# Layer 1 of a three-stage kernel: seven token tiles, three of them 512 wide, in place of eight of 384

## Chip, cores and metric

One Trainium2 chip, one NeuronCore. The time is that of one execution on the device in microseconds, the median of the runs shown; lower is better. A profile of one execution gives the trace.

## What is computed

A gated linear attention with a state per head, then two feed-forward layers over the same 3072 tokens (4 batches of 768), all in float32.

```python
for t in range(S):                      # B, H, S, D = 4, 8, 768, 48
    state = alpha[:, :, t, :, None] * state + einsum('bhd,bhe->bhde', k[:, :, t], v[:, :, t])
    y[:, :, t] = einsum('bhd,bhde->bhe', q[:, :, t], state)
x = y.transpose(0, 2, 1, 3).reshape(B * S, H * D)                  # 3072 x 384
x = (1 / (1 + exp(-(x @ w_gate))) * (x @ w_val)) @ w_out           # layer 1, d_ff 1536
out = maximum(maximum(x @ w1, x @ w2), x @ w3) @ w_out2            # layer 2, d_ff 768
```

## The kernel before

The program is written by hand for each engine, with semaphores between them; each engine runs its instructions in the order written.

**Layer 1** goes over tiles of tokens (`TOK` = 384, `TILES` = 8). Within a tile it goes over the 12 blocks of 128 hidden features, here called steps f = 0 to 11. A step on TensorE is `layer1` (line 1069): the gate product (`product`, lines 1020 and 1026), the value product, and the output product of the step before (`out1`, line 1045). For float32 accuracy each operand is split in a high and a low part and three of the four cross products are taken, so each of these is 3 x 3 = 9 matmuls of 128 x 128 weights against a moving operand as wide as the tile: 27 matmuls a step. ScalarE makes the sigmoid of the gate bank (`act_sb`, line 491) and the high part of h (`h_hi`, line 445), VectorE multiplies (`h_sb`, line 791) and makes the low part (`h_lo`, line 753). TensorE waits for the sigmoid before it writes the gate bank again, for h before the value bank.

**Attention** goes over 24 chunks of 128 tokens (`CH`). The first three are made ahead of layer 1; those of the tile T + 1 are made between the steps of tile T. For a chunk, VectorE runs scans of the decay factors alpha (`scans`, line 674, `decay`) and, after a reciprocal at each half chunk's end, reverse scans (`recips`, line 689, `rdec`); GpSimd scales queries and keys (`scale_qk`, lines 411 and 415); TensorE makes scores and transposes (lines 947 and 926), then outer products for the state (`outer`, line 961), and in the next step the values (`attend`, lines 994 and 976). VectorE masks the scores (`masked`, line 701), makes the next state (`new_state`, lines 724 to 729) and adds the crossed blocks (`y_add`, line 743); ScalarE copies keys (`khs_copy`), outputs (`y_copy`, line 445, into `x_raw`) and checks the range of alpha (lines 554 and 561). From the second tile on GpSimd scales; in the first, VectorE does.

The steps are fixed in the code: scans at f = 0, 3 and 6, scores at 2, 5 and 8, values at 3, 6 and 9, additions at 4, 7 and 9. On VectorE:

```python
if att and f % 3 == 0 and not scanned:
    scans(*att)
elif att and f % 3 == 2:
    masked(*att, 0)
    masked(*att, 1)
```

Before the scores TensorE waits for the last chunk's addition (`y_added`), before the outer products for both masks (`mask_done`) and the copied keys.

**Loads.** SP loads each chunk in two transfers: alpha (256 KB, line 281) and then queries, keys and values (704 KB, line 285), into one of two buffers by the chunk's parity. A buffer is free when the chunk two before has been attended and checked (`y_done`, `viol_done`). When all chunks of a tile are added, SP moves rows of the last heads into place (`move_last`, line 312). ScalarE and VectorE then split the tile's inputs (`x_hi`, `x_lo`) in step 11, for the next tile.

**Layer 2** has six tiles of 512 tokens and six steps of three products of 512 columns (27 matmuls) and an output product of 12 matmuls of 384 columns (line 1140). TensorE's layer 1 is written out tile by tile; ScalarE, VectorE, GpSimd and SP run tiles 1 to 6 in a hardware loop of two tiles a pass, three passes, so that semaphore counts are computed from a register.

## Time and profile before

| | us |
|---|---|
| median of 3 runs (850.42 to 850.93) | 850.75 |
| the profiled execution | 850.66 |
| span of its trace | 848.6 |
| TensorE busy | 838.0 |
| VectorE, ScalarE, GpSimd busy | 389.0, 280.2, 74.5 |

The span runs from the first instruction to the last end on the core; the execution's own time has some 2 us around it. Busy times of TensorE count pipelined matmuls as overlapping, so the starts tell more than the durations. The profile names a group of instructions by its line, its engine and the names it writes and reads. The rows that matter are in a section of their own below.

### The profile page before, as it was taken

How to read it: one execution, taken by the hardware profiler on the slowest of the kernel's cores; microseconds unless marked ns; L12 is line 12 of the kernel's file. 1: busy time of each engine (PE TensorE's matmuls, PEld its weight loads, DVE VectorE, ACT ScalarE, POOL GpSimd, SP SyncE). 2: the span in 40 equal slices, each digit the busy share in tenths (PEclk: the TensorE clock that was granted, in tenths of full speed). 3: DMA queues.
4: the chain of work that ended last, by engine and by line, in shares of the span. 5: the costliest groups of instructions: out<-in, count | busy, mean ns of one | idle time of the engine just before them, and what ended most of it. 6: DMA issues, size and time to landing. Idle time of an engine off the chain costs nothing.

```text
span 848.6 us, 17210 instructions
## 1 busy us (share of the span) xinstructions
PE 838.0 (99%) x6997; PEld 773.5 (91%) x6997; DVE 389.0 (46%) x959; ACT 280.2 (33%) x520; POOL 74.5 (9%) x68
## 2 busy tenths in 40 slices
PE   8999999999999999999999999999999999999997
PEld 7899999999999999999999999988888888888886
DVE  8787565555555455466465322323223232232321
ACT  4655333333333333333333334322212122221212
POOL 1000111111111011021021006300000000000000
PEclk9999999999999999999999999999999999999999
DMA  7440210210210210210200103100101001010101
GB/s 287 163 181 3 100 48 2 101 48 2 101 47 2 100 48 2 101 47 2 100 27 23 49 34 113 38 1 0 38 1 37 0 0 37 0 37 0 37 0 39
DMA packets 14461, 42.36 MB, mean 50 GB/s; under 512 B 1984, under 2 KB 5952, under 8 KB 14400
## 3 DMA queue, kind: packets, MB, share of 16 engines
q1 hardware_dynamic: 14336, 41.41, 13.7%
q8 instruction: 49, 0.80, 0.4%
q14 instruction: 12, 0.10, 0.0%
q10 hardware_dynamic: 64, 0.05, 0.0%
HBM read 35.56 MB, written 4.72 MB: 47 GB/s over the span
## 4 chain that ended last, share of the span: by engine, by line
PE 96%; DVE 2%; DMA 1%; issue 1%; ACT 0%; SPq 0%; DVEq 0%
PE ps_gv L1020 35%; PE ps_out L1045 19%; PE ps_gv L1026 18%; PE ps_out L1140 6%; PE ps_sc L1020 6%; PE ps_sc L1026 3%; PE ps_pair L1140 2%; PE ps_pair L994 1%; PE ps_pair L976 1%; PE ps_pair L926 1%; PE ps_sc L947 1%; PE ps_sc L961 1%; PE ps_pair L947 1%; DVE decay L674 0%; DVE rdec L689 0%
## 5 line engine op out<-in xcount | busy, mean ns | idle before, releaser
L1020 PE MATMUL ps_gv<-x_hi,w_hi 128*128 128x384 f32 (+1 forms) x792 | 279.8, 353 | 1.1 <-ACT x_hi L445 1.1
L1020 PE MATMUL ps_gv<-x_hi,w_lo 128*128 128x384 f32 (+1 forms) x792 | 277.2, 350 | 0.0
L1026 PE MATMUL ps_gv<-x_lo,w_hi 128*128 128x384 f32 (+1 forms) x792 | 235.1, 351 | 0.0
L1020 PEld LDWEIGHTS ps_gv<-x_hi,w_hi 128*128 128x128 f32 x792 | 148.8, 188 | 9.6 <-ACT w_hi L445 1.3
L1020 PEld LDWEIGHTS ps_gv<-x_hi,w_lo 128*128 128x128 f32 x792 | 148.9, 188 | 7.5
L1026 PEld LDWEIGHTS ps_gv<-x_lo,w_hi 128*128 128x128 f32 x792 | 146.0, 188 | 9.6
L791 DVE TENSOR_TENSOR h_sb<-act_sb,ps_gv 128x384 f32<-128x384 f32 x96 | 53.2, 554 | 145.7 <-PE ps_gv L1026 145.4
L445 ACT ACTIVATE h_hi<-h_sb 128x384 fp32r<-128x384 f32 x96 | 50.3, 524 | 145.9 <-DVE h_sb L791 145.8
L491 ACT ACTIVATE act_sb<-ps_gv 128x384 f32<-128x384 f32 x96 | 47.2, 491 | 137.0 <-PE ps_gv L1026 137.0
L890 DVE TENSOR_TENSOR probs<-probs,ps_gv 128x512 f32<-128x512 f32 x36 | 24.8, 689 | 137.9 <-PE ps_gv L1026 137.9
L753 DVE TENSOR_TENSOR h_lo<-h_sb,h_hi 128x384 fp32r<-128x384 f32 x96 | 54.3, 566 | 52.0 <-ACT h_hi L445 52.0
L1045 PE MATMUL ps_out<-h_hi,w_hi 128*128 128x384 f32 x288 | 70.1, 351 | 0.0
L445 ACT ACTIVATE h_hi<-probs 128x512 fp32r<-128x512 f32 x36 | 22.8, 632 | 130.4 <-DVE probs L894 130.3
L1045 PE MATMUL ps_out<-h_hi,w_lo 128*128 128x384 f32 x288 | 65.4, 335 | 0.0
L1045 PE MATMUL ps_out<-h_lo,w_hi 128*128 128x384 f32 x288 | 65.4, 334 | 0.0
L689 DVE TENSOR_TENSOR_SCAN rdec<-inbuf,rdec,zero 112x63 f32<-112x63 f32 (+1 forms) x176 | 54.5, 381 | 0.8
L411 POOL TENSOR_TENSOR inbuf<-inbuf,decay 112x512 f32<-112x512 f32 x18 | 23.1, 1285 | 341.2 <-DVE decay L674 341.2
L1045 PEld LDWEIGHTS ps_out<-h_hi,w_hi 128*128 128x128 f32 x288 | 48.8, 188 | 2.9
L1045 PEld LDWEIGHTS ps_out<-h_hi,w_lo 128*128 128x128 f32 x288 | 51.4, 188 | 0.0
L1045 PEld LDWEIGHTS ps_out<-h_lo,w_hi 128*128 128x128 f32 x288 | 51.3, 188 | 0.0
L445 ACT ACTIVATE probs<-ps_gv 128x512 f32<-128x512 f32 x36 | 21.5, 598 | 81.2 <-PE ps_gv L1026 81.2
L894 DVE TENSOR_TENSOR probs<-probs,ps_sc 128x512 f32<-128x512 f32 x36 | 24.7, 687 | 48.6 <-PE ps_sc L1026 48.6
(128 smaller groups left out, 971.4 us busy)
## 6 DMA issues: line engine op xcount, KB each, us to landing
inbuf<-att_in SPq DMA_DIRECT2D x23, 704.0 KB, 4.5
mid<-w SPq DMA_DIRECT2D x12, 576.0 KB, 7.3
inbuf<-att_in SPq DMA_DIRECT2D x23, 256.0 KB, 3.1
inbuf<-w SPq DMA_DIRECT2D x6, 768.0 KB, 4.3
out<-inbuf SPq DMA_DIRECT2D x5, 768.0 KB, 3.5
x_raw<-x_raw SPq DMA_DIRECT2D x46, 24.0 KB, 1.9
out<-inbuf SPq DMA_DIRECT2D x4, 192.0 KB, 2.9
mid<-att_in SPq DMA_DIRECT2D x1, 704.0 KB, 9.1
```

What stands on the lines that cost most here:

```text
L411: nc.gpsimd.tensor_tensor(att(buf(Cs), Q), att(buf(Cs), Q), decay[0:PR, par], ALU.mult).then_inc(qh_done, 1)
L445: return nc.scalar.activation(o, i_, ACT.Copy)
L491: nc.scalar.activation(act_sb[:, :], ps_gate[:, 0:TOK], ACT.Sigmoid).then_inc(sig_done, 1)
L689: nc.vector.tensor_tensor_scan(rdec[0:PR, par, p, lo:hi][:, ::-1], att(buf(Cs), ALPHA)[:, p, lo + 1:hi + 1][:, ::-1], zero[0:PR, :].broadc ...
L753: nc.vector.tensor_tensor(h_lo[:, f % 2, 0:w], h, h_hi[:, f % 2, 0:w].bitcast(F32), ALU.subtract).then_inc(lo_done, 1)
L791: nc.vector.tensor_tensor(h_sb[:, :], act_sb[:, :], ps_val[:, 0:TOK], ALU.mult).then_inc(h_done, 1)
L890: nc.vector.tensor_tensor(act2, act2, ps_val[:, :], ALU.max).then_inc(ab_done, 1)
L894: nc.vector.tensor_tensor(h2, act2, ps_sc[:, :], ALU.max).then_inc(h2_done, 1)
L1020: mm(bank, w_at(half, f, c + k * P, total=total), x_hi[:, k, 0:w], start=(k == 0 and half == 0), stop=False)
L1026: return mm(bank, w_at(0, f, c + k * P, total=total), x_lo[:, k, 0:w], start=False, stop=(k == KT - 1))
L1045: ins = mm(ps_out[:, m, 0:TOK], w_at(wh, f, 2 * DM + m * P), h[:, f % 2, 0:TOK], start=(f == 0 and n == 0), stop=(f == NF1 - 1 and n == 2))
L1140: ins = mm(out_bank[s][:, 0:DM], h[:, f % 2, s * P:(s + 1) * P], w_at(wh, f, 3 * DM, DM, W2C), start=(f == 0 and n == 0), stop=(f == NF2 - ...
```

## The change

`SIZES` sets the tiles of layer 1: four of 384 tokens and three of 512. `THREE` and `FOUR` hold the steps at which the chunks of the next tile are scanned, scored and added: four chunks for tiles 4, 5 and 6 (prepared in tiles 3, 4 and 5), the first of them scanned in step 10 of the tile before (-2). With four chunks a scan and a score share steps 4 and 6, and a value product and an addition share steps 5, 7 and 9. Buffers that were 384 columns wide have 512. `rdec` has one buffer instead of two, so `recips` waits for the keys of the chunk before. On VectorE `new_state` now precedes `recips`. SP loads the first chunk of the tile after next ahead of the moves of the last heads. The loops of SP, GpSimd, ScalarE and VectorE over tiles are written out. What a step computes is unchanged.

```diff
-TILES = B * S // TOK
+SIZES = (384, 384, 384, 384, 512, 512, 512)
+TILES = len(SIZES)
+START = tuple(sum(SIZES[:T]) for T in range(TILES + 1))
+FIRST = tuple(t // CH for t in START)
+PRO = FIRST[1]
+THREE = {"scan": (0, 3, 6), "score": (2, 5, 8), "add": (4, 7, 9)}
+FOUR = {"scan": (-2, 2, 4, 6), "score": (1, 4, 6, 8), "add": (3, 5, 7, 9)}
+STEPS = (THREE, THREE, THREE, FOUR, FOUR, FOUR)
...
-        act_sb = sb("act_sb", [P, TOK])
-        h_sb = sb("h_sb", [P, TOK])
+        act_sb = sb("act_sb", [P, TOK2])
+        h_sb = sb("h_sb", [P, TOK2])
...
-        rdec = sb("rdec", [P, 2, PAIRS, CH])
+        rdec = sb("rdec", [P, PAIRS, CH])
...
+        def chunk_at(T, f, what):
+
+            for tile, step in ((T, f), (T + 1, f - NF1)):
+                at = STEPS[tile][what] if tile < len(STEPS) else ()
+                if step in at:
+                    return FIRST[tile + 1] + at.index(step)
+            return None
...
-            load_chunk(5, 0)
-            move_last(1)
-            with sp.Fori(0, (TILES - 2) // 2) as i:
-                for Ts in (1, 2):
-                    for c in range(CPT):
-                        load_chunk(CPT * (Ts + 1) + c, i)
-                    move_last(Ts + 1 + 2 * i, past=Ts + 2 * i)
+            load_chunk(5)
+            for T in range(1, TILES - 1):
+                load_chunk(FIRST[T + 1])
+                move_last(T)
+                for C in range(FIRST[T + 1] + 1, FIRST[T + 2]):
+                    load_chunk(C)
+            move_last(TILES - 1)
...
-                    if not (isinstance(i, int) and Cs < 2):
-                        dve.wait_ge(kh_done, 2 * C - 2)
...
+                    if C > 0:
+                        dve.wait_ge(kh_done, 2 * C)
...
-                    c = f // 3
-                    att = (C0 + c, i) if att_next and c < CPT else None
-                    scanned = first and c == 0
-                    if att and f % 3 == 0 and not scanned:
-                        scans(*att)
-                    elif att and f % 3 == 2:
-                        masked(*att, 0)
-                        masked(*att, 1)
+                    scanned, scored, added = (chunk_at(T, f, steps) for steps in ("scan", "score", "add"))
+                    if scanned == PRO:
+                        scanned = None
+                    if scanned is not None:
+                        scans(scanned)
+                    if scored is not None:
+                        masked(scored, 0)
+                        masked(scored, 1)
...
-                    if att and f % 3 == 0 and not scanned:
-                        recips(*att, range(PAIRS))
-                    if att and f % 3 == 2:
-                        new_state(*att)
-                    if att_next and not first and f in (4, 7, 9):
-                        y_add(C0 + (4, 7, 9).index(f), i)
+                    if scored is not None:
+                        new_state(scored)
+                    if scanned is not None:
+                        recips(scanned, range(PAIRS))
+                    if added is not None and crossed(added):
+                        y_add(added)
...
-                    product(ps_gate[:, 0:TOK], f, 0, W1C, T * KT if f == 0 else None).then_inc(gate_done, 1)
-                    if att_next and f in (2, 5, 8):
-                        scores(C0 + (f - 2) // 3, i)
-                        transposes(C0 + (f - 2) // 3, i)
+                    product(ps_gate[:, 0:w], f, 0, W1C, T * KT if f == 0 else None).then_inc(gate_done, 1)
+                    scored, attended = chunk_at(T, f, "score"), chunk_at(T, f - 1, "score")
+                    if scored is not None:
+                        scores(scored)
+                        transposes(scored)
```

Two places show what moves. The first is VectorE's order in tile 3, from the addition of a chunk in step 5 to the next states in step 6 (`L766` adds, `L699` scans, `L725` masks, `L813` and `L777` are h and its low part, `L750` and `L752` the state):

```order
278 L766 TENSOR_TENSOR x_raw<-x_raw,ps_pair 48x2x64 [waits y_evac]
279 L766 TENSOR_TENSOR x_raw<-x_raw,ps_pair 48x2x64 x3
280 L699 SCALAR_TENSOR_TENSOR decay<-inbuf,zero 112x64 [waits rdec_done,state_done,qh_done,alpha_loaded1]
281 L699 SCALAR_TENSOR_TENSOR decay<-inbuf,zero 112x64 x7
282 L725 TENSOR_TENSOR probs<-ps_sc,cst 128x256 [waits y_done,sc_done]
283 L725 TENSOR_TENSOR probs<-ps_pair,cst 128x256 [waits sc_done]
284 L813 TENSOR_TENSOR h_sb<-act_sb,ps_gv 128x384 [waits h_lo_done,sig_done,val_done]
285 L777 TENSOR_TENSOR h_lo<-h_sb,h_hi 128x384 [waits h_hi_done]
286 L750 TENSOR_TENSOR stmp<-ps_sc,state 112x192 [waits state_done,y_done,u_done]
287 L752 TENSOR_TENSOR state<-stmp,decay 112x192 [waits stmp_done]
```

In the kernel before, the addition is followed by the masks alone (the same names at their old lines, tile 1 of the loop):

```order
153 L743 TENSOR_TENSOR x_raw<-x_raw,ps_pair 48x2x64 [waits y_evac]
154 L743 TENSOR_TENSOR x_raw<-x_raw,ps_pair 48x2x64
155 L741 COPY x_raw<-ps_pair 48x2x64 x2
156 L701 TENSOR_TENSOR probs<-ps_sc,cst 128x256 [waits y_done,sc_done]
157 L701 TENSOR_TENSOR probs<-ps_pair,cst 128x256 [waits sc_done]
158 L788 REGISTER_ALU
159 L791 TENSOR_TENSOR h_sb<-act_sb,ps_gv 128x384 [waits h_lo_done,sig_done,val_done]
```

The scans of the next chunk, which wait for its alpha, have moved in between the addition and the masks.

The second is SP's queue around the end of a tile (`L310` and `L314` load a chunk, `L342` moves the last heads), here with the four chunks of tile 4:

```order
39 L342 DMA x_raw<-x_raw 16x384 [waits y_added,y_evac]
40 L342 DMA x_raw<-x_raw 16x384 x5
41 L310 DMA inbuf<-att_in 128x512 [waits viol_done,y_done]
42 L314 DMA inbuf<-att_in 128x1408
43 L310 DMA inbuf<-att_in 128x512 [waits viol_done,y_done]
44 L314 DMA inbuf<-att_in 128x1408
45 L310 DMA inbuf<-att_in 128x512 [waits viol_done,y_done]
46 L314 DMA inbuf<-att_in 128x1408
47 L310 DMA inbuf<-att_in 128x512 [waits viol_done,y_done]
48 L314 DMA inbuf<-att_in 128x1408
49 L342 DMA x_raw<-x_raw 16x512 [waits y_added,y_evac]
50 L342 DMA x_raw<-x_raw 16x512 x5
```

Rows 41 to 46 are the last three chunks of tile 4, rows 47 and 48 the first chunk of tile 5, which now stands ahead of tile 4's moves (rows 49 and 50) instead of behind them.

## Rows read from the trace of the kernel before

**Rows 1.** Engine totals of the page, and TensorE's granted clock in 40 slices.
```profile
PE 838.0 (99%) x6997; PEld 773.5 (91%) x6997; DVE 389.0 (46%) x959; ACT 280.2 (33%) x520; POOL 74.5 (9%) x68
...
PEclk9999999999999999999999999999999999999999
```
**Rows 2.** The chain that ended last, by engine.
```profile
PE 96%; DVE 2%; DMA 1%; issue 1%; ACT 0%; SPq 0%; DVEq 0%
```
**Rows 3.** TensorE's waits, longest of six: who, for whom, us, times, longest.
```profile
PE ps_sc L947 <- DVE inbuf L770: 1.7, 1, 1.7
```
**Rows 4.** Timeline of TensorE (start us, us, engine, line, what); windows' sums of layer 1.
```profile
290.49 0.33 PE L1020 MATMUL ps_gv<-x_hi,w_hi 128*128 128x384 f32 x1
...
295.24 0.34 PE L1020 MATMUL ps_gv<-x_hi,w_hi 128*128 128x384 f32 x1
...
299.92 0.33 PE L1020 MATMUL ps_gv<-x_hi,w_hi 128*128 128x384 f32 x1
...
27.66:544.46 516.80, 515.63 (x5309) 493.33 (x5309) 281.94 (x779) 201.59 (x382) 70.74 (x60) 1.00 0.17 60
```
**Rows 5.** Timeline of TensorE, a step of layer 2.
```profile
701.02 0.39 PE L1020 MATMUL ps_gv<-x_hi,w_hi 128*128 128x512 f32 x1
...
703.10 0.39 PE L1020 MATMUL ps_gv<-x_hi,w_hi 128*128 128x512 f32 x1
...
707.18 0.33 PE L1140 MATMUL ps_out<-w_hi,h_hi 128*128 128x384 f32 x1
```
**Rows 6.** Timeline of TensorE, steps 2 to 5 of tile 4: firsts of groups.
```profile
301.57 0.27 PE L947 MATMUL ps_sc<-inbuf 48*64 48x64 f32 x1
...
304.31 0.25 PE L961 MATMUL ps_sc<-inbuf,khs 64*48 64x48 f32 x2
...
306.49 0.33 PE L1020 MATMUL ps_gv<-x_hi,w_hi 128*128 128x384 f32 x1
...
312.42 0.33 PE L1020 MATMUL ps_gv<-x_hi,w_hi 128*128 128x384 f32 x1
...
317.10 0.34 PE L1020 MATMUL ps_gv<-x_hi,w_hi 128*128 128x384 f32 x1
...
318.89 0.24 PE L947 MATMUL ps_sc<-inbuf 48*64 48x64 f32 x1
```
**Rows 7.** Timeline of VectorE, the same steps.
```profile
306.04 0.35 DVE L727 TENSOR_TENSOR stmp<-ps_sc,state 112x192 f32<-112x192 f32 x1
...
307.49 1.56 DVE L674 TENSOR_TENSOR_SCAN decay<-inbuf,zero 112x64 f32<-112x64 f32 x8
...
311.44 0.20 DVE L684 RECIPROCAL rdec<-decay 112x8 f32<-112x8 f32 x1
311.67 2.52 DVE L689 TENSOR_TENSOR_SCAN rdec<-inbuf,rdec,zero 112x63 f32<-112x63 f32 x8
315.74 0.56 DVE L791 TENSOR_TENSOR h_sb<-act_sb,ps_gv 128x384 f32<-128x384 f32 x1 [1.55 <-PE ps_gv L1026]
316.88 0.56 DVE L753 TENSOR_TENSOR h_lo<-h_sb,h_hi 128x384 fp32r<-128x384 f32 x1 [0.59 <-ACT h_hi L445]
317.36 1.17 DVE L743 TENSOR_TENSOR x_raw<-x_raw,ps_pair 48x128 f32<-48x128 f32 x4
319.65 0.42 DVE L701 TENSOR_TENSOR probs<-ps_sc,cst 128x256 f32<-128x256 f32 x1 [1.11 <-PE ps_pair L947]
```
**Rows 8.** A chunk's loads on SP (issue; KB, us to landing), and GpSimd's last key product.
```profile
311.05 0.33 SPq L281 DMA_DIRECT2D inbuf<-att_in  x1
...
inbuf<-att_in SPq DMA_DIRECT2D x1, 704.0 KB, 5.5
inbuf<-att_in SPq DMA_DIRECT2D x1, 256.0 KB, 3.4
...
314.27 0.74 POOL L415 TENSOR_TENSOR inbuf<-inbuf,rdec 112x256 f32<-112x256 f32 x1 [0.71 <-DVE rdec L689]
```
**Rows 9.** DMA issues of the page: the transfers of layer 1's weights.
```profile
mid<-w SPq DMA_DIRECT2D x12, 576.0 KB, 7.3
```

More of the change, by code:

```diff
@@ L164, in v_cols, with tile_of, chunks_of, x_of @@
             return buf_cols(b, ATT + lo, n)
[L166 to L175 removed]
+        def tile_of(C):
+            return next(T for T in range(TILES) if C in chunks_of(T))
+        def chunks_of(T):
+            return range(FIRST[T], FIRST[T + 1]) if T < TILES else range(0)
+        def chunk_at(T, f, what):
[4 more added lines that the diff above has]
+            return None
+        def x_of(T, k):
+            return x_raw[:, k, 0:SIZES[T]] if T < TILES else mid_tile2(0, k)
+        def tr_bank(C):
+            if C < PRO:
+                return ps_sc if C == 1 else ps_out[:, 1, :]
+            return ps_tr
+        def outer_bank(C, s):
+            if C < PRO:
+                return tr_bank(C)[:, 0:PAIRS * D]
             return (ps_sc, ps_sc_odd)[s][:, 0:PAIRS * D]
[L178 to L180 removed]
+        def y_banks(C):
+            two = ps_gv if C == 1 else ps_pair
             return two[:, 512 - 2 * CH:512 + 2 * CH].rearrange("p (s t) -> p s t", s=PAIRS)
[L183 to L185 removed]
+        def crossed(C):
+            return C >= FIRST[2]
         def cross_bank(s):
@@ L428, in _ @@
             split_first(2).then_inc(w_lo_done, 1)
-            with pool.Fori(0, (TILES - 2) // 2) as i:
-                for Ts in (1, 2):
-                    for c in range(CPT):
-                        scale_qk(CPT * (Ts + 1) + c, i)
+            for C in range(FIRST[2], CHUNKS):
+                scale_qk(C)
             for j in range(NF2):
@@ L508, in layer1 @@
+                    attended = chunk_at(T, f - 1, "score")
+                    if attended is not None:
+                        y_copy(attended)
+                    if scored is not None:
+                        check(scored)
                     if f == NF1 - 1:
                         for k in range(1, KT):
-                            if att_next:
+                            if n_next:
                                 act.wait_ge(last_moved[k], 32 * T + 64)
-                            x_split(T + 1, k, *((x_raw[:, k, :],) if att_next else (mid_tile2(0, k), TOK2)))
@@ L612, in split_w2 @@
                 return go
-            layer1(TILES - 1, 0, False, True, {LAST_READ[j] + 2: split_w2(j) for j in range(NF2)})
+            layer1(TILES - 1, {LAST_READ[j] + 2: split_w2(j) for j in range(NF2)})
             def o_copy_last():
@@ L715, in next_state @@
-            def next_state(Cs, i, s):
-                j = state_at(Cs, i, s)
-                past = states_by(Cs, i) - subs(Cs, i) + s
+                for s in range(subs(C)):
+                    next_state(C, s)
+            def next_state(C, s):
+                j = state_at(C, s)
+                past = states_by(C) - subs(C) + s
                 old, new = state[0:PR, j], state[0:PR, (j + 1) % 3]
-                u = outer_bank(Cs, i, s)[0:PR, :].rearrange("p (a e) -> p a e", a=PAIRS)
-                last = span_of(Cs, i, s).stop - 1
-                end = decay[0:PR, Cs % 2, :, last:last + 1].broadcast_to([PR, PAIRS, D])
-                if Cs % (2 * CPT) == 0 and s == 0:
+                u = outer_bank(C, s)[0:PR, :].rearrange("p (a e) -> p a e", a=PAIRS)
+                last = span_of(C, s).stop - 1
+                end = decay[0:PR, C % 2, :, last:last + 1].broadcast_to([PR, PAIRS, D])
+                if C % BATCH == 0 and s == 0:
@@ L949, in scores, with outer @@
                 ins.then_inc(sc_done, 1)
-            def outer(Cs, i):
-                C, par = Cs + 6 * i, Cs % 2
+            def outer(C):
+                par = C % 2
                 pe.wait_ge(khs_done, C + 1)
-                if not (isinstance(i, int) and Cs < CPT):
+                if C >= PRO:
                     pe.wait_ge(mask_done, 2 * C + 2)
                 for p in range(PAIRS):
-                    for s in range(subs(Cs, i)):
-                        t = span_of(Cs, i, s)
+                    for s in range(subs(C)):
+                        t = span_of(C, s)
@@ L996, in attend @@
                                start=(p < 2 and s == (1 if first else 0)), stop=False, skip_group_check=True)
-                if subs(Cs, i) == 1:
+                if subs(C) == 1:
                     for p in range(PAIRS):
                         for n in range(2):
-                            ins = value(Cs, i, p, n, 0, start=(first and p < 2))
+                            ins = value(C, p, n, 0, start=(first and p < 2))
                 else:
```

605 lines of the change are left out of this document (289 added, 316 removed).

## The prediction

> **What bounds the kernel now.** I read the engine totals first. TensorE is busy for 838.0 us of a span of 848.6 us, VectorE for less than half of it, and TensorE's granted clock is in the top tenth in every slice, that is 2.4 GHz throughout [rows 1]. The chain of work that ended last is 96% TensorE [rows 2]. TensorE's own waits are six events, none longer than 1.7 us [rows 3]. A busy share can hide stalls between pipelined matmuls, so I took starts, not durations. A step of layer 1 without attention work (27 matmuls over 384 columns) starts at 295.24 us and the next at 299.92 us [rows 4]: 4.68 us, or 173.3 ns a matmul, although one "takes" 340 ns. Layer 1 runs from 27.66 to 544.46 us [rows 4], 516.8 us. So TensorE's issue time is the bound, and other engines count only where they make TensorE start late.
>
> **What a matmul costs by its width.** Layer 2 has the width that the change brings. Its value product and its third product (18 matmuls of 512 columns) go from 703.10 to 707.18 us [rows 5]: 226.7 ns each. From 384 to 512 columns the price rises by 53.3 ns, which is 128 columns at 2.4 GHz; 384 columns at that clock are 160.0 ns. So each matmul of either width pays 13.3 ns on top of its columns.
>
> **The sum, part by part.**
> 1. *Fewer, wider matmuls.* Layer 1 issues 27 matmuls in each of 12 steps of a tile: 8 x 12 x 27 = 2592 of 384 columns now; after the change 4 x 12 x 27 = 1296 stay, and the other 1296 become 3 x 12 x 27 = 972 of 512. 1296 x 173.3 = 224.6 us, 972 x 226.7 = 220.3 us: **-4.3 us**. All of it is on TensorE's chain. The columns are the same; 324 fixed parts go. The Trainium skill (TensorE: Matmul & The Clock Gate, on the gap of 56 ns) puts the fixed part of a warm matmul at about 2.5 ns; by that the term would be 324 x 2.5 = 0.8 us, and the trace disagrees with it, with 13.3 ns at both widths.
> 2. *One tile boundary less.* The first step of a tile takes 290.49 to 295.24 us, 4.75 us instead of 4.68 [rows 4]: **-0.07 us**.
> 3. *A small wait that the wider tiles cover.* The first score product of a tile starts 1.65 us after its step (299.92 to 301.57), the next one 1.79 us after (317.10 to 318.89) [rows 6]. What differs is that VectorE has just finished adding the crossed blocks (317.36 + 1.17 = 318.53 us [rows 7]), for which the scores wait; add to start is 0.36 us. Twelve score products wait so now (two in each of tiles 1 to 6, 0.14 us each). In the 512-wide tiles the gate product is nine matmuls x 53.3 = 0.48 us longer, and the add is over before: six are left (two each in tiles 1, 2 and 3), **-0.84 us**.
> 4. *Four chunks of attention in tile 3.* This is the tight place: it has 384 columns but prepares four chunks, and scans and scores fall into the same step, 4 and 6. Work first: scans 1.56, two masks of 0.42 that overlap a little, 0.8, the gate product h 0.56, ScalarE's turn 0.59, h_lo 0.56, the two states 1.5, reciprocal and reverse scans 0.20 + 2.52 + 0.03 [rows 7] make 8.3 us on VectorE, more than the step's 6.7 us. The next step asks for 2.9 us, so the pair needs 11.2 us and has 6.7 (306.49 - 299.92 and item 3) + 5.9 (312.42 - 306.49, the step with the value products) = 12.6 us [rows 6]. It fits, and the keys, 2 x 0.74 us on GpSimd behind the scans [rows 8], are ready some 3 us before the next scores. What does come late is the load of the decay factors for the fourth chunk. Its buffer is free when the second has been attended, 4.5 us into step 5 (311.05 - 306.49 [rows 6, 8]); it lands 3.4 us later, 2.0 us into step 6; scans end at 3.65 us, the masks at 4.4, and with 0.36 us to TensorE the outer products start at 4.8 instead of 4.39 + 0.14 us (304.31 - 299.92 [rows 6], and the wait of item 3): **+0.3 us**. The queries and keys of that chunk land 5.5 us after their issue [rows 8], about 4.7 us into step 6, in time for step 8. VectorE is 0.5 us late with h of step 5, which TensorE wants only in step 6.
> 5. *The same in tiles 4 and 5.* At 512 columns a step is 27 x 53.3 ns = 1.44 us longer. The load is then issued 4.5 + 2 x 0.48 = 5.5 us into a step 5 of 5.93 + 1.44 = 7.4 us and lands 1.5 us into step 6; scans and masks are done at 3.9 us, seen by TensorE at 4.3, and the outer products come at 4.39 + 0.96 = 5.35 us: 1.1 us to spare, **0**.
> 6. *Rest of the path, 0 each.* Attention is still 24 chunks with the same matmuls. The splits at tile ends have a third more columns, but the output product that covers them grows by a third too, by 0.48 us. The first chunk's load now stands ahead of the moves of the last heads on SP; its condition (the chunk before the last attended) holds earlier than that of the moves (the last one added), so the moves lose nothing, and the chunk gains a tile's end. A single reciprocal buffer makes the next reciprocals wait for the keys of the chunk before; these precede that chunk's scores, which in every row of steps stand ahead of the reciprocals. The loops written out take register instructions from VectorE, ScalarE, GpSimd and SP, none of which has the chain.
>
> Sum: -4.3 - 0.07 - 0.84 + 0.3 = **-4.9 us**, from the profiled execution's 850.66 us to **845.8 us**. It lies 0.09 us under the median shown, 850.75, so the two references are the same here. What this kernel's measurement can tell from no change I take as 0.2%, 1.7 us.
>
> **Bounds of what the trace does not show.** No 512-column product follows a 512-column output product in layer 1 yet. The nearest rows speak for two prices: the gate product of layer 2 takes 701.02 to 703.10 us [rows 5], 231.1 ns a matmul, and the two after it 226.7. If it is the product itself that is dear and not its following a 384-column one, 324 matmuls x 4.4 ns = 1.4 us come back. In layer 1 the gate product after an output product of its own width shows nothing of the kind (4.68 us for all 27), so I take 0 and keep 1.4 us as the upper end. For item 4 the lower end is 0 (no stall), the upper 1 us (the late h and the late add meet in the scores of steps 6 and 8, 0.2 to 0.4 us each). Item 3 lies between 0 and 12 x 0.14 = 1.7 us of gain.
>
> **Rivals.**
> - *The price goes by columns* (chance 0.10). Then 512 columns cost 173.3 x 4/3 = 231.1 ns, exactly what layer 2's gate product shows [rows 5], on all 972 matmuls. Item 1 is gone, items 2 to 4 leave 850.0 us: no change. Against it: 18 of the 27 wide matmuls of each layer 2 step are at 226.7. The small fixed part in the Trainium skill (same page and section as above) would end at almost the same place; with item 1 at 0.8 us it gives 849.3 us.
> - *VectorE holds up the outer products in all four-chunk tiles* (0.06), the case on the other side. Place: step 6 of tiles 3, 4 and 5, where the scans of the fourth chunk stand ahead of the masks in VectorE's order, so masks that could run wait behind scans that wait for a transfer. The price hangs on the landing. With 3.4 us it is item 4. If it landed as late as the median weight transfer, 7.3 us [rows 9], tile 3 would lose 0.3 + 3.9 = 4.2 us and tiles 4 and 5 3.9 - 1.1 = 2.8 us each: 9.8 us instead of 0.3, 855.3 us. The gain is gone from a landing of 5.8 us on (2.4 us later than in the rows: 2.4 + 2 x 1.3 = 5.0). Against it: nothing else moves on the queues then, and the load is 256 KB like all the others.
> - *The four-chunk steps leak a little everywhere* (0.12): the upper ends above together, +1.4 (gate) + 0.7 (tile 3) + 0.8 (item 3 gives nothing): 848.7 us, still faster, by 0.24%.
> - Forecast, 844.9 to 847.8 us: 0.72.
>
> **From this the numbers.** Faster by over 0.2% (under 849.0 us) are the forecast and most of the leak: 0.83. Same: the price by columns and the rest of the leak, 0.11. Slower: 0.06. The range goes from 844.8 us (item 3 at its best, no stall in tile 3) to 848.7 us, the leak's end; outside are the by-columns case, the rival on the other side and some of the leak.
>
> **What would show it.** In the changed profile: matmuls of 512 columns in layer 1 spaced 227 ns (a plain step of tile 6 of 6.12 us, of tiles 0 to 3 still 4.68); layer 1 of 511.4 us instead of 516.8, and layer 2 0.5 us longer than 304.1, since the last tile's nine output products lie behind its start; in tile 3, step 6, outer products about 0.3 us late; the second to fourth scores of tiles 4 and 5 with no extra 0.14 us; TensorE's waits still six of at most 1.7 us. I am wrong if plain steps in tiles 4 to 6 take over 6.2 us (price by columns: 6.24), or if tile 5 is over 86.5 us (12 x 6.12 = 73.4, and four times 1.89 for the step with scores and 1.25 for that with value products, from [rows 6], make 86.0; what is above is a stall that I did not see).

## The result, and the profile after

| | before | after | |
|---|---|---|---|
| median, us | 850.62 (850.42 to 850.93, 4 runs) | 843.92 (843.83 to 843.99, 4 runs) | ratio 0.9921, 95% interval 0.9909 to 0.9933 |
| the profiled execution | 850.66 | 843.96 | -6.70 |
| span of its trace | 848.63 | 842.16 | -6.47 |

The change makes the kernel 6.7 us faster. The forecast was 4.9 us, with a range that ends at 844.8 us; the time lies below it. The direction was right, the size was not.

The page of the changed kernel looks like the one before [rows 1, 2]: TensorE 99% busy, clock in the top tenth throughout, a chain of TensorE alone.

```profile
PE 834.4 (99%) x6673; PEld 731.6 (87%) x6673; DVE 384.4 (46%) x932; ACT 274.6 (33%) x490; POOL 74.4 (9%) x68
...
PEclk9999999999999999999999999999999999999999
...
PE 97%; DVE 2%; DMA 1%; issue 1%; ACT 0%; SPq 0%; DVEq 0%
```

TensorE's waits are again six, none over 1.7 us; the longest (who, for whom, us, times, longest; compare [rows 3]). Nothing here says where 6.7 us went, because the waits in question are hidden among pipelined matmuls, and the end of the program is no wait of TensorE.

```profile
PE ps_out L1117 <- POOL state L447: 1.4, 1, 1.4
```

So the span is cut at four starts: the first gate product, the first product of layer 2, the last matmul, the end. The windows view of the changed kernel, tile by tile (the first two numbers are the stretch and its us; then busy us and instructions of TensorE, its weight loads, VectorE, ScalarE and GpSimd, the clock, the DMA share and GB/s):

```profile
27.61:539.05 511.44, 510.75 (x4985) 450.36 (x4985) 277.42 (x752) 196.09 (x353) 70.65 (x60) 1.00 0.18 61
...
224.79:293.47 68.68, 68.60 (x838) 64.72 (x837) 43.95 (x134) 27.17 (x55) 11.04 (x12) 1.00 0.19 61
293.47:379.19 85.72, 85.72 (x838) 68.82 (x837) 47.50 (x134) 30.14 (x56) 11.04 (x12) 1.00 0.15 50
379.19:465.45 86.26, 86.26 (x853) 69.19 (x852) 43.77 (x118) 30.22 (x56) 8.27 (x9) 1.00 0.14 45
465.45:539.05 73.60, 73.60 (x327) 60.82 (x325) 18.84 (x30) 26.29 (x38) 20.96 (x6) 1.00 0.13 43
539.05:838.83 299.78, 299.63 (x1414) 259.68 (x1412) 85.75 (x126) 64.03 (x115) 0.00 (x0) 1.00 0.04 13
838.83:842.16 3.33, 0.34 (x2) 0.01 (x1) 0.00 (x0) 0.83 (x2) 0.00 (x0) 1.00 0.67 239
```

The last two stretches of the kernel before, for comparison (its layer 1 is in [rows 4]):

```profile
544.46:843.88 299.42, 299.27 (x1414) 259.64 (x1413) 85.69 (x126) 63.96 (x115) 0.00 (x0) 1.00 0.04 13
843.88:848.63 4.75, 0.34 (x2) 0.01 (x1) 0.00 (x0) 0.83 (x2) 0.00 (x0) 0.89 0.50 173
```

| stretch | before | after | difference | forecast |
|---|---|---|---|---|
| up to the first gate product | 27.66 | 27.61 | -0.05 | 0 |
| layer 1 | 516.80 | 511.44 | -5.36 | -5.4 |
| layer 2, up to the last matmul | 299.42 | 299.78 | +0.36 | +0.5 |
| from the last matmul to the end | 4.75 | 3.33 | **-1.42** | 0 |
| outside the span | 2.03 | 1.80 | -0.23 | 0 |

Up to the last matmul the forecast holds: -5.05 us where the sum said -4.9. What is missing from it is the end. (The prediction's own sign for layer 2 and the end together was 0.5 us more than 304.1; they came out at 303.1.)

**The end of the program.** In both kernels SP stores four blocks of the output there. The timeline of the kernel before has all four in one row (start, us), and narrow windows of it part them:

```profile
843.25 2.77 SPq L397 DMA_DIRECT2D out<-inbuf  x4
...
843.73 0.35 SPq L397 DMA_DIRECT2D out<-inbuf  x1
...
843.73 1.81 SPq L397 DMA_DIRECT2D out<-inbuf  x2
...
845.59 0.43 SPq L397 DMA_DIRECT2D out<-inbuf  x1
```

The second takes 0.35 us, the second and third together 1.81 with a pause of 0.17 between them: the third, issued at 844.25, takes 1.29 us, and the last stands behind it. After the change, with the stores on other lines of the program:

```profile
838.20 1.85 SPq L427 DMA_DIRECT2D out<-inbuf  x4
...
839.20 0.33 SPq L427 DMA_DIRECT2D out<-inbuf  x1
```

Here the third takes 0.33 us like the others. The last store is issued 0.89 us after the last matmul's start instead of 1.71, which is 0.8 of the 1.4 us; the other 0.6 us is that it lands 2.0 us after its issue instead of 2.6. (The second store lands late too before the change, 3.2 us after its issue instead of 1.9, although its issue takes no longer; whether the fetch holds up transfers as well as issues stays open.) The DMA view names a candidate. The last 9 us of the kernel before have a packet of a queue that carries instructions, 16 KB, which starts at 843.88 and takes 1.28 us (8.0% of 16 engines in the view of 843 to 844 us); the last 8 us of the changed kernel have none. Queue q14 also has one packet more before the change; in the sixth experiment it has both packets and the end is short, so it is not the cause.

```profile
q8 instruction: 1, 0.02, 0.9%
q14 instruction: 2, 0.02, 0.7%
...
q8 instruction: 1, 0.02, 8.0%
```

```profile
q14 instruction: 1, 0.01, 0.4%
```

After the last tile of layer 2 TensorE passes over the code of a branch that is not taken here (a slow version of the computation, for decay factors out of range) to the few instructions behind it. If these lie in a part of the program that it does not hold yet, they are fetched, at the very time of the stores. Whether the fetch is what lengthens SP's issue was then an open question; it has experiments of its own below (the sixth to the eighth).

### The profile page after: what moved, and what is told of

It is laid out like the page before. It is cut to its first block, busy times and chain, and to the rows that moved or that the text cites. A ratio compares the mean times of both kernels' runs of the same rounds, so it can differ in the third digit from the quotient of the medians.

```text
span 842.2 us, 15966 instructions
## 1 busy us (share of the span) xinstructions
PE 834.4 (99%) x6673; PEld 731.6 (87%) x6673; DVE 384.4 (46%) x932; ACT 274.6 (33%) x490; POOL 74.4 (9%) x68
## 4 chain that ended last, share of the span: by engine, by line
PE 97%; DVE 2%; DMA 1%; issue 1%; ACT 0%; SPq 0%; DVEq 0%
PE ps_gv L1039 35%; PE ps_out L1063 19%; PE ps_gv L1045 18%; PE ps_out L1155 6%; PE ps_sc L1039 6%; PE ps_sc L1045 3%; PE ps_pair L1155 2%; PE ps_pair L1013 1%; PE ps_pair L995 1%; PE ps_pair L946 1%; PE ps_sc L966 1%; PE ps_sc L980 1%; PE ps_pair L966 0%; DVE rdec L714 0%; DVE decay L699 0%
## 5 line engine op out<-in xcount | busy, mean ns | idle before, releaser
L1039 PE MATMUL ps_gv<-x_hi,w_hi 128*128 128x512 f32 (+1 forms) x720 | 267.1, 371 | 1.1 <-ACT x_hi L473 1.1
L1039 PE MATMUL ps_gv<-x_hi,w_lo 128*128 128x512 f32 (+1 forms) x720 | 264.7, 368 | 0.0
L1045 PE MATMUL ps_gv<-x_lo,w_hi 128*128 128x512 f32 (+1 forms) x720 | 226.2, 368 | 0.0
L813 DVE TENSOR_TENSOR h_sb<-act_sb,ps_gv 128x384 f32<-128x384 f32 (+1 forms) x84 | 51.2, 610 | 149.2 <-PE ps_gv L1045 149.2
L473 ACT ACTIVATE h_hi<-h_sb 128x384 fp32r<-128x384 f32 (+1 forms) x84 | 48.0, 571 | 146.5 <-DVE h_sb L813 146.1
L517 ACT ACTIVATE act_sb<-ps_gv 128x384 f32<-128x384 f32 (+1 forms) x84 | 45.1, 537 | 142.4 <-PE ps_gv L1045 142.4
L777 DVE TENSOR_TENSOR h_lo<-h_sb,h_hi 128x384 fp32r<-128x384 f32 (+1 forms) x84 | 51.7, 615 | 49.1 <-ACT h_hi L473 49.1
L1063 PE MATMUL ps_out<-h_hi,w_hi 128*128 128x384 f32 (+1 forms) x252 | 67.9, 377 | 0.0
L1063 PE MATMUL ps_out<-h_hi,w_lo 128*128 128x384 f32 (+1 forms) x252 | 63.2, 358 | 0.0
L1063 PE MATMUL ps_out<-h_lo,w_hi 128*128 128x384 f32 (+1 forms) x252 | 63.0, 358 | 0.0
```

The source lines that it names most:

```text
L473: return nc.scalar.activation(o, i_, ACT.Copy)
L517: nc.scalar.activation(act_sb[:, 0:w], ps_gate[:, 0:w], ACT.Sigmoid).then_inc(sig_done, 1)
L777: nc.vector.tensor_tensor(h_lo[:, f % 2, 0:w], h, h_hi[:, f % 2, 0:w].bitcast(F32), ALU.subtract).then_inc(lo_done, 1)
L813: nc.vector.tensor_tensor(h_sb[:, 0:w], act_sb[:, 0:w], ps_val[:, 0:w], ALU.mult).then_inc(h_done, 1)
L1039: mm(bank, w_at(half, f, c + k * P, total=total), x_hi[:, k, 0:w], start=(k == 0 and half == 0), stop=False)
L1045: return mm(bank, w_at(0, f, c + k * P, total=total), x_lo[:, k, 0:w], start=False, stop=(k == KT - 1))
```

## The experiments

**1. All that the change does, but the widths.** The changed kernel with the old tiles:

```diff
-SIZES = (384, 384, 384, 384, 512, 512, 512)
+SIZES = (384,) * 8
...
-STEPS = (THREE, THREE, THREE, FOUR, FOUR, FOUR)
+STEPS = (THREE,) * 7
```

> The changed kernel with eight tiles of 384 again (SIZES eight times 384, steps THREE in all seven); written-out programs, the single reciprocal buffer and the new order on SP stay. Theory (the width is the gain): layer 1 is as long as before the change, 516.8 us from the first gate product to layer 2, within 0.2 us, with twelve score products 0.14 us late; the whole lies at 850.6 us if the last stores of the output again meet a 16 KB instruction fetch, at 849.2 us if not. Rival (the written-out programs or SP's order carry a part): layer 1 gets shorter than 516.8 us by 0.5 us or more, and the whole comes under 849 us.

Measured: 850.05 us (849.70 to 850.51, 10 runs) beside 850.75 (19 runs), ratio 0.9993 (0.9983 to 1.0003). Layer 1 is as it was:

```profile
27.70:544.40 516.70, 515.49 (x5309) 493.64 (x5310) 281.68 (x779) 202.41 (x382) 70.89 (x60) 1.00 0.18 60
```

Its third store is again a long one (1.67 us), beside a 16 KB fetch that starts at 843.84, and its end takes 4.88 us. So the fetch is there with all loops written out, as long as TensorE has the old tiles. By the median, the loops written out, the new order on SP and the single reciprocal buffer can't be told from no change; all of the gain in layer 1 and at the end belongs to the widths. One small part does not: outside the span this kernel has 1.8 us in each of its ten runs and the changed kernel 1.8 to 1.9, while the kernel before has 2.0 to 2.2.

**2. The wait of item 3 alone.** The kernel before, with each addition a step earlier where it stood in the step ahead of the scores:

```diff
-                    if att_next and not first and f in (4, 7, 9):
-                        y_add(C0 + (4, 7, 9).index(f), i)
+                    if att_next and not first and f in (3, 6, 9):
+                        y_add(C0 + (3, 6, 9).index(f), i)
```

> The kernel before, with the crossed blocks of a chunk added in steps 3, 6 and 9 instead of 4, 7 and 9, nothing else. Theory (TensorE's score products wait for that addition, 0.36 us after its end): the twelve score steps of 6.71 to 6.73 us become 6.57 us, 12 x 0.14 = 1.7 us less, 848.9 us. Rival (the 0.14 us is something else of the second and third score product of a tile, such as more semaphores to look at): the steps stay at 6.7 us and the whole at 850.6 us; a third outcome, that the earlier addition makes VectorE late for h and the value product, would show as steps 4 and 7 over 4.68 us.

Measured: 849.08 us (848.66 to 850.25, 10 runs), ratio 0.9982 (0.9972 to 0.9991), 1.67 us less. Layer 1 falls by 1.66 us, layer 2 stays:

```profile
27.74:542.88 515.14, 514.82 (x5308) 492.99 (x5309) 281.69 (x779) 201.62 (x382) 70.74 (x60) 1.00 0.17 60
542.88:842.30 299.42, 299.26 (x1414) 259.53 (x1413) 85.58 (x126) 63.95 (x115) 0.00 (x0) 1.00 0.04 13
```

1.66 us over twelve score products is 0.14 us each. The mechanism and the price of item 3 are shown.

**3. The same in the changed kernel.**

```diff
-THREE = {"scan": (0, 3, 6), "score": (2, 5, 8), "add": (4, 7, 9)}
-FOUR = {"scan": (-2, 2, 4, 6), "score": (1, 4, 6, 8), "add": (3, 5, 7, 9)}
+THREE = {"scan": (0, 3, 6), "score": (2, 5, 8), "add": (3, 6, 9)}
+FOUR = {"scan": (-2, 2, 4, 6), "score": (1, 4, 6, 8), "add": (2, 5, 7, 9)}
```

> The changed kernel, with the additions at steps 3, 6, 9 (three chunks) and 2, 5, 7, 9 (four chunks). Five score products still wait 0.14 us in the changed kernel (two each in tiles 1 and 2, one in tile 3). Theory: they stop, 5 x 0.14 = 0.7 us less than the changed kernel's 843.9 us, 843.2 us. Rival (the wait is something else): 843.9 us. If the addition right behind the reverse scans of the same step were late for the next h, it would be above 843.9 us.

Measured: 843.30 us (843.23 to 843.33, 4 runs), ratio to the kernel before 0.9913 (0.9897 to 0.9930). It is the fastest version of the study, some 0.6 us under the changed kernel. One score product shows it, in step 5 of tile 2. In the changed kernel (a step begins with the first row, the addition ends at 186.90, the scores start at 187.25):

```profile
185.46 0.33 PE L1039 MATMUL ps_gv<-x_hi,w_hi 128*128 128x384 f32 x1
...
187.25 0.24 PE L966 MATMUL ps_sc<-inbuf 48*64 48x64 f32 x1
```

```profile
185.72 1.18 DVE L766 TENSOR_TENSOR x_raw<-x_raw,ps_pair 48x128 f32<-48x128 f32 x4
```

In this version no addition stands there, and the scores start 1.66 us into the step instead of 1.79:

```profile
185.18 0.33 PE L1039 MATMUL ps_gv<-x_hi,w_hi 128*128 128x384 f32 x1
...
186.84 0.27 PE L966 MATMUL ps_sc<-inbuf 48*64 48x64 f32 x1
```

**4. The masks ahead of the scans.** The rival on the other side rests on the scans standing ahead of the masks. So they change places:

```diff
-                    if scanned is not None:
-                        scans(scanned)
                     if scored is not None:
                         masked(scored, 0)
                         masked(scored, 1)
+                    if scanned is not None:
+                        scans(scanned)
```

> The changed kernel with the masks ahead of the scans on VectorE in steps 4 and 6 of tiles 3, 4 and 5. Theory (nothing in those steps waits for the masks; the last mask ends 3.83 us or less into the step and the outer products come at 4.40 us or later): same time as the changed kernel, 843.9 us, within 0.2 us. Rival (the scans ahead of the masks hold up the outer products a little in places): up to 0.5 us faster. If the later scans make the queries and keys late for the next scores: slower, with score steps over 6.57 and 8.06 us.

Measured: 844.21 us (844.13 to 844.43, 4 runs), ratio to the kernel before 0.9924 (0.9908 to 0.9941). No gain, and 0.3 us over the changed kernel where the theory allowed 0.2: the scans held nothing up. Tile 3 even takes 68.82 us instead of 68.68, because scans that come later push the additions behind them, and those of steps 6 and 8 then end late enough (1.33 and 1.37 us into the step instead of 1.13) to delay the scores by 0.03 and 0.08 us.

**5. The price of a matmul by its width.** The changed kernel with the gate and value products of its last tile (no attention beside them) narrowed step by step; the columns left out are not computed, and the output product stays at 512:

```diff
-                w = SIZES[T]
                 for f in range(NF1):
+                    w = SIZES[T] if T < TILES - 1 or f in (0, 11) else (512, 512, 448, 448, 384, 320, 256, 192, 128, 512, 512, 512)[f]
```

> The changed kernel, where the gate and value products of the last tile of layer 1 go over fewer columns: steps 1 to 8 over 512, 448, 448, 384, 320, 256, 192 and 128; the left-out columns of the gate and value banks keep what the step before left there, so part of layer 1's last tile isn't computed. Output products stay at 512 columns. Theory (a fixed 13.3 ns on top of the columns at 2.4 GHz): matmul to matmul in the value product 200.0 ns at 448, 173.3 at 384, 146.7 at 320, 120.0 at 256, 93.3 at 192, 66.7 at 128, unless a floor from loading the weights shows. Rival (the price goes by columns, 0.4427 to 0.4513 ns each): 198 to 202 at 448, 142 to 144 at 320, 113 to 116 at 256, 85 to 87 at 192, 57 to 58 at 128. For the dear first product after narrower ones: the output product (512) after narrower gate and value products should show 228 to 236 ns in its first matmuls, and 227 in step 1, where all are 512 wide.

One run, 834.95 us. The rows of the step with 320 columns, from the value product (nine matmuls) over the output product (nine of 512 columns, three to a row) to the next gate product:

```profile
495.84 0.31 PE L1039 MATMUL ps_gv<-x_hi,w_hi 128*128 128x320 f32 x1
...
497.16 0.86 PE L1063 MATMUL ps_out<-h_hi,w_hi 128*128 128x512 f32 x3
497.86 0.85 PE L1063 MATMUL ps_out<-h_hi,w_lo 128*128 128x512 f32 x3
498.55 0.84 PE L1063 MATMUL ps_out<-h_lo,w_hi 128*128 128x512 f32 x3
499.23 0.28 PE L1039 MATMUL ps_gv<-x_hi,w_hi 128*128 128x256 f32 x1
```

497.16 - 495.84 = 1.32 us, 146.7 ns a matmul; 320 columns at 2.4 GHz are 133.3. The value products of the other steps, read the same way:

| columns | 512 | 448 | 384 | 320 | 256 | 192 | 128 |
|---|---|---|---|---|---|---|---|
| ns from start to start | 226.7 | 203 | 173.3 | 146.7 | 120 | 112 | 112 |
| columns at 2.4 GHz | 213.3 | 186.7 | 160.0 | 133.3 | 106.7 | 80.0 | 53.3 |

From 512 down to 256 columns the difference is 13.3 ns (16 at 448), so the price is not one by columns: that would be 144.4 ns at 320 and 115.6 at 256. Below 256 columns a floor of some 112 ns takes over. What sets it no run shows; the weight load that stands beside each matmul is a candidate. The output rows show a second effect: nine 512-wide matmuls behind narrower ones take 2.07 us, 230 ns each, the first three 233 and the last three 227; behind 512-wide ones they take 226.7 throughout.

**6. The fetch moved, in the kernel before.** 88 increments of a semaphore that nobody waits for, ahead of TensorE's loop of layer 2, move the code behind them along in the program:

```diff
             layer2(0, lambda: out1(TILES - 1, 0, NF1 - 1))
+            for _ in range(88):
+                pe.sem_inc(spare, 1)
```

> The kernel before, with 88 increments of a spare semaphore in TensorE's program ahead of layer 2's loop, nothing else; they move where 16 KB pages of the program end. Theory (the last stores of the output are issued late because TensorE's jump to the end of its program enters a new page and starts a 16 KB instruction fetch, which the third store's issue meets): the fetch at 843.9 us is gone or comes before the first store, the third issue takes 0.33 us instead of 1.29, and the stretch from the last matmul to the end is 3.3 us instead of 4.7: 849.3 us. Rival (the late issue comes from SP's own program or from the transfers themselves): the issue still takes 1.3 us and the time stays at 850.7 us. If the increments themselves hold up TensorE, its start of layer 2's second tile moves and the time is above 850.7 us.

Measured: 862.16 us (861.03 to 863.42, 4 runs), ratio 1.0138 (1.0121 to 1.0155). The time itself says nothing, because the increments cost far more than expected: where they stand, TensorE issues nothing for 10 us, and the two steps there take 11.9 us more (18.70 and 9.73 instead of 8.27 each). The second of them has no pause: it is long because TensorE's granted clock fell to half, 1.2 GHz, while the engine issued nothing, and came back only in the course of that step (0.84 in its mean), which its first matmul shows with 0.79 us instead of 0.39. So the increments' own price is the 10.4 us of the first step, and the clock's 1.5 us come on top.

```profile
603.91 0.79 PE L1021 MATMUL ps_gv<-x_hi,w_hi 128*128 128x512 f32 x1 [10.27 <-issue]
...
603.91:613.64 9.73, 9.72 (x39) 8.33 (x40) 1.89 (x3) 1.23 (x2) 0.00 (x0) 0.84 0.00 0
```

The end answers nevertheless. The fetch is now at 854.62, before the first store at 855.07, and none of the four issues is long (0.34, 0.41, 0.39, 0.35):

```profile
855.07 1.86 SPq L398 DMA_DIRECT2D out<-inbuf  x4
```

The end takes 3.31 us instead of 4.75, as after the change. The same kernel, the same stores; but for the increments only the place of the fetch differs. That the packet moves when TensorE's program alone is edited, here and in the next two experiments, also shows whose instructions it carries.

**7. A fetch at the end of the changed kernel.** 100 matmuls that are never executed, in the branch not taken:

```diff
                 pe.sem_inc(s2_out, 1)
                 pe.wait_ge(s_mid, SLOW_TILES * KT + KT)
+                for _ in range(100):
+                    mm(ps_sc[:, 0:CH], ident, ident, start=True, stop=True)
                 with pe.Fori(0, TILES2) as T:
```

> The changed kernel, with 100 more matmuls in TensorE's branch for out-of-range inputs, which isn't taken: only the end of its program lies 200 instructions further on. Theory (the jump over that branch enters a new page and the fetch meets the stores): a 16 KB fetch near 838.8 us, an issue of a store of over 1 us instead of 0.33, a tail of 4.7 us instead of 3.3, and 845.3 us instead of 843.9. Rival (the tail's length has to do with something else in the written-out programs): 843.9 us.

Measured: 846.46 us (845.58 to 847.93, 4 runs; the profiled one 845.58), ratio to the kernel before 0.9954 (0.9937 to 0.9971). Layer 2 starts at 539.05 as before the edit. The second store is now the long one, and the fetch is back:

```profile
838.19 3.25 SPq L427 DMA_DIRECT2D out<-inbuf  x4
...
838.65 1.82 SPq L427 DMA_DIRECT2D out<-inbuf  x1
```

```profile
q8 instruction: 2, 0.03, 1.6%
```

It starts at 838.72 and takes 1.38 us; the second fetch of this window, at 842.9, comes after the stores' issues. The end takes 4.97 us instead of 3.33: 1.64 us for code that does not run. Two of the four runs are another 2 us longer; only one run was profiled, so why stays open.

**8. A fetch by a shift of the changed kernel.** 170 increments at the same place as in the sixth:

```diff
             layer2(0, lambda: out1(TILES - 1, NF1 - 1))
+            for _ in range(170):
+                pe.sem_inc(spare, 1)
```

> The changed kernel, with 170 increments of a spare semaphore in TensorE's program ahead of layer 2's loop, so that a 16 KB page ends between the loop and the end of the program, as in the kernel before. Theory: as in the run with the longer branch, a fetch near the last stores and 845.3 us; should the page end before the last products, the fetch can come before the stores, and then it is 843.9 us with a fetch at 837 us or earlier. Rival: 843.9 us with no change in the stores' issues.

Measured: 870.37 us (869.12 to 872.38, 4 runs), ratio 1.0237 (1.0220 to 1.0254). Again the increments cost more than all else: the two steps take 31.15 and 9.74 us, 24.3 more, of which the second step's 1.5 us are the clock again. The fetch starts at 863.16 and is shorter (0.88 us), the third issue takes 0.83 us, and the end 4.10 us, between the two cases. It agrees in sign, and adds that the issue takes about as long as the fetch lasts (0.83 us for a fetch of 0.88; 1.29 for 1.28 in the kernel before, 1.67 for 1.64 in the first experiment, 1.10 for 0.98 in the second, but 1.82 for 1.38 in the seventh).

**9. The price of a late landing.** The rival on the other side, brought about: for the chunks of tiles 3 to 6, SP loads queries, keys and values first, and alpha behind them.

```diff
-                load_alpha(C)
-                load_qkv(C)
+                if C > FIRST[2]:
+                    sp.wait_ge(y_done, C - 1)
+                    sp.wait_ge(viol_done, C - 1)
+                    load_qkv(C)
+                    load_alpha(C)
+                else:
+                    load_alpha(C)
+                    load_qkv(C)
```

> The changed kernel, with each later chunk's queries, keys and values (704 KB) loaded ahead of its alpha (256 KB) instead of behind, so that alpha lands some 2 us later. It prices the rival of the prediction in which the scans ahead of the masks hold up the outer products. Theory, from the changed kernel's trace: in step 6 of tile 3 the load is issued 1.5 us before the step and alpha then lands 4.6 us after that, at 3.1 us; scans and masks are done at 5.5, the outer products start at 5.8 us instead of 4.40, +1.4 us; in tiles 4 and 5 alpha lands at 3.0 us of step 6, masks are done at 5.4, the outer products start at 5.75 instead of 5.38 us, +0.35 us each: 2.1 us in all, 846.0 us, and no other step changes. Rival (the changed kernel has more slack there than the ledger says, or the two transfers share the engines so that both land together at 4.2 us): under 845 us.

Measured: 845.80 us (845.54 to 846.14, 4 runs) beside 850.67, ratio 0.9943 (0.9926 to 0.9959); layer 1 takes 513.52 us, 2.08 more than the changed kernel's. Step 6 of tile 3 starts at 259.20. Its scans wait for the load, and the outer products for the masks behind them:

```profile
262.52 1.57 DVE L705 TENSOR_TENSOR_SCAN decay<-inbuf,zero 112x64 f32<-112x64 f32 x8 [2.18 <-DMA inbuf<-att_in]
264.12 0.42 DVE L731 TENSOR_TENSOR probs<-ps_sc,cst 128x256 f32<-128x256 f32 x1
264.46 0.41 DVE L731 TENSOR_TENSOR probs<-ps_pair,cst 128x256 f32<-128x256 f32 x1
```

```profile
265.02 0.25 PE L986 MATMUL ps_sc<-inbuf,khs 64*48 64x48 f32 x2 [1.35 <-DVE probs L731]
```

The outer products start 5.82 us into the step instead of 4.39, and it takes 7.99 us instead of 6.57: +1.42. In tile 5 the same step takes 8.67 instead of 8.06 (+0.61), in tile 4 nothing is lost. The theory had the total and tile 3 right. Tiles 4 and 5 add up to it only by luck: it had put 0.35 us on each. In tile 4 alpha lands 4.2 us after its issue; in tile 5 the load meets a 16 KB fetch (from 421.73, 1.30 us), its issue takes 1.16 us and it lands after 5.0. The masks' end reaches TensorE within 0.15 us (264.87 to 265.02). So the rival's mechanism is real: scans that wait for alpha hold up the outer products. Its conditions are further off than the prediction put them.

## Why the prediction was off

**Item 1, fewer and wider matmuls: right.** Three successive steps of the last tile, of 6.12 us each, are 226.7 ns a matmul:

```profile
465.45 0.39 PE L1039 MATMUL ps_gv<-x_hi,w_hi 128*128 128x512 f32 x1
...
471.57 0.39 PE L1039 MATMUL ps_gv<-x_hi,w_hi 128*128 128x512 f32 x1
...
477.69 0.39 PE L1039 MATMUL ps_gv<-x_hi,w_hi 128*128 128x512 f32 x1
```

324 fixed parts of 13.3 ns are the 4.3 us, and the fifth experiment shows that the part is fixed over other widths too. The rival by columns has fallen, and so has the time worked out beside it from the small fixed part in the Trainium skill (TensorE: Matmul & The Clock Gate, Wait — 56ns, not 53.3ns?).

**Item 2, the tile boundary: right in kind, 0.3 us instead of 0.07.** It is not one boundary less of 0.07 us: only the first steps of 384-wide tiles cost 0.03 to 0.07 us more than a plain one, seven of them before and three now; those of tiles 5 and 6 take 6.12 us like all the others.

**Item 3, the small wait: the mechanism right, one too few.** Seven waits vanish instead of six, 1.0 us instead of 0.84: tile 3 keeps one (step 4), not two, since its additions in steps 6 and 8 end 1.13 us into the step, where the scores would start at 1.66. I had carried the rows of a three-chunk tile over to a tile with another order.

**Item 4, the tight step of tile 3: wrong, 0 instead of +0.3 us.** This is it in the changed kernel; the step starts at 259.11, SP issues the load of alpha at 257.59:

```profile
259.04 1.18 DVE L766 TENSOR_TENSOR x_raw<-x_raw,ps_pair 48x128 f32<-48x128 f32 x4 [0.53 <-ACT x_raw L473]
260.25 1.56 DVE L699 TENSOR_TENSOR_SCAN decay<-inbuf,zero 112x64 f32<-112x64 f32 x8
261.85 0.42 DVE L725 TENSOR_TENSOR probs<-ps_sc,cst 128x256 f32<-128x256 f32 x1
262.19 0.41 DVE L725 TENSOR_TENSOR probs<-ps_pair,cst 128x256 f32<-128x256 f32 x1
```

```profile
263.50 0.25 PE L980 MATMUL ps_sc<-inbuf,khs 64*48 64x48 f32 x2
```

The load lands before the addition is over, and the scans follow that without a gap. The masks end at 262.60, 0.9 us before the outer products, which start at their usual 4.39 us. Two numbers were too large. The 3.4 us of landing were taken from one load [rows 8], and it was not a typical one: a 16 KB fetch of instructions ran into the same chunk's transfers, and the issue behind it took 1.74 us where 0.33 is usual.

```profile
311.05 0.33 SPq L281 DMA_DIRECT2D inbuf<-att_in  x1
311.57 1.74 SPq L285 DMA_DIRECT2D inbuf<-att_in  x1
...
q8 instruction: 1, 0.02, 7.0%
```

(the last line is the DMA view of 311.4 to 312.6 us). In the other five of tiles 1 to 6 the load at the same place landed after 2.6 to 3.1 us. The median over all chunks would have hidden this: it is 3.3 us in the kernel before, because the second load of each tile is issued right behind the first and lands late (4.4 to 5.9 us). In the changed kernel the load of the tight step is there by 2.5 us, and the median is 2.8. And from masks to TensorE I took the 0.36 us measured from an addition to the scores, where the ninth experiment shows 0.15. The earlier landing alone takes the 0.3 us away; the shorter way alone would have taken 0.2 of it.

**Item 5, right:** the outer products of tiles 4 and 5 are on time. **Item 6, right** as far as layer 1 goes: the first experiment puts the rest of the change within the measurement's uncertainty. The end of the path, which item 6 passed over, is the step that failed, below.

**A cost that I had set at 0.** The bound on the gate product was taken in full or not at all. It is the following of a wider matmul on narrower ones that costs. In layer 1 this happens after every insertion of attention work: a score step of a 512-wide tile takes 8.06 us, 1.94 more than a plain one (I had 1.89), a step with values 7.39, 1.27 more (1.25). With the first 512-wide step (5.73 instead of 5.64) that is some 0.7 us in all. In return the first gate product of layer 2, now behind output products of its own width, is no longer dear (0.1 us). Tile 5 so takes 86.26 us, against the 86.0 worked out and the alarm at 86.5.

These add up to -4.3 - 0.3 - 1.0 + 0.7 - 0.1 = -5.0 us; measured to the last matmul are -5.05. That the sum came out so close, at -4.9, is in part luck: items 2, 3 and 4 together came out 0.7 us lower than forecast, and the surcharge of 0.7 us offset them.

**The step that failed is the rest of the path, put at 0, and with it the sum's frame.** The sum started from the whole profiled time, 850.66 us, and let only TensorE's chain change; item 6, "Rest of the path, 0 each", has no word on what follows the last matmul. The end had no term. It had one of 1.4 us: a 16 KB fetch that met the third store. With 324 matmuls and their weight loads fewer, TensorE's code has come to lie otherwise, and the fetch no longer falls into the last 8 us. The loops written out for the other engines are not the reason, since the first experiment has them and the fetch as well. The sixth experiment takes it away from the kernel before (-1.4 us at the end), the seventh gives it back to the changed one (+1.6).

The Trainium skill (Runtime: NRT & Kernel Launch, Instruction fetch mechanics) says that instructions come in blocks of 16 KiB, and that a taken branch to outside the two blocks held forces a fetch of its target before execution can go on. The fetch at 843.88 us, when TensorE starts its last matmul, with the jump over the branch still to come, agrees, and so does the seventh experiment, where code that never runs brings a fetch. By the Trainium skill the stall would be TensorE's, which has nothing left to do here; in the traces it is SP that pays. The one long issue in four, beside the fetch, stood in the trace of before. Whether the fetch would go does not follow from the diff, but a bound of -1.4 us would have put 843.9 us inside the range. (The range's lower end was also added up wrongly: 845.8 less 0.3 and 0.86 is 844.6 us, not 844.8. The time lies below both.)

The last 0.23 us lie outside the span. They come with the other parts of the change and not with the widths, as the first experiment shows; which part, and why, stays open.

**The rival on the other side** was priced by 9.8 us for a landing of 7.3, with the gain gone at 5.8. By the ninth experiment tile 3 starts to lose when alpha's data come over 3.4 us after the issue (2.66 us plus the 0.75 to spare), tile 5 from about 4.9 (scans up to 2.9 us into the step cost nothing, and the load is issued 2.0 us ahead of it). By an estimate from these numbers the gain of 6.7 us would be gone at some 6.6 us, if tile 4 is like tile 5. In the changed kernel the three loads in question landed after 2.5, 2.6 and 2.9 us, and no load of alpha in tiles 3 to 5 took more than 3.7.

## What to carry to other kernels

Cut a span at the starts of the bounding engine, head and tail included, and give each piece a term or a bound, even the microseconds after the last matmul: a store's issue there is on the path, and whether an instruction fetch meets it depends on how long the code is, the code that never runs too. Before a single row serves as a price, look at whether its neighbours were disturbed, and compare it with the row at the same place of other tiles; the median of a mixed group can look just like the disturbed row. Where matmuls are the bound and other engines have room, fewer and wider ones gain their fixed part, 13.3 ns each here, and small waits of 0.14 us at fixed places are found by offsets from the start of the step, not by the list of waits.

## What was not expected of the hardware

- A 16 KB fetch of instructions for TensorE can stretch a DMA issue on SP that overlaps it, from 0.33 to 0.59 us to 0.8 to 1.8 us. Eleven such meetings stand in the two traces (0.82 to 1.74 us), more at the ends of four experiments (0.83 to 1.82). Not every issue that overlaps a fetch is stretched: at 843.73 us before the change and at 113.71 and 196.58 after it, one kept its usual 0.33 to 0.43. At a program's end the fetch costs 0.8 to 1.6 us.
- An increment of a semaphore on TensorE that nobody waits for is not free: 88 of them stop TensorE's matmuls for 10.3 us, 170 for 22.7, some 0.15 us for each of the 82 more. In the pause the granted clock falls to 1.2 GHz, which costs another 1.5 us behind it.
- A 512-wide matmul behind narrower ones mostly takes 228 to 236 ns instead of 226.7, for the next 4 to 9 matmuls.
- Below 256 columns, with a new weight tile for each, a matmul does not get cheaper: some 112 ns at 192 and at 128.
